# A fused attention, gated-FFN and mixture-of-experts kernel: weight blocks, clip order, score copies and filler products of the opening slots rearranged

## What is computed

```python
# attention: batch 2, 8 heads, 576 rows, head size 64
scores = scale * q @ k.T
kth = the 32nd largest of each row;  scores = where(scores >= kth, scores, -1e9)
attn = exp(scores - max) / (sum + 1e-9);  x = attn @ v          # -> 1152 x 512
# gated FFN, 512 -> 1536 -> 512
xn = x / rms(x) * rms_g;  g = xn @ w_gate
x = (g * sigmoid(g) * (xn @ w_val)) @ w_out
# experts: softmax gate over 8, argmax, capacity 288
y = relu(x_e @ w1[e]) @ w2[e];  out = gate * y
```

## Time and profile before

| | us |
|---|---|
| three executions | 663.43, 663.98, 665.63 |
| median | 663.98 |
| profiled execution, its own time | 665.63 |
| its span, first to last instruction | 663.8 |

### The profile page before, as it was taken

The page is one execution under the profiler, slowest core; times in us unless marked ns, Lnnn a source line. Parts: engine busy times, 40 slices in busy tenths (PEclk is TensorE's granted clock), DMA queues, the critical chain, the costliest instruction groups (busy, mean ns, idle before and its releaser), DMA issues.

```text
span 663.8 us, 11121 instructions
## 1 busy us (share of the span) xinstructions
PE 617.8 (93%) x3934; PEld 475.5 (72%) x3934; DVE 418.2 (63%) x915; ACT 326.3 (49%) x713; POOL 258.6 (39%) x361
## 2 busy tenths in 40 slices
PE   7777879999999999999999999999999999999994
PEld 5444555675775775775775775766769999999994
DVE  3999899799699699798898897931111110111110
ACT  3575884774865865766756756753211111111100
POOL 1284884454544544555455364462310101111101
PEclk9987999999999999999999999999999999999998
DMA  9999300000010010000000000000197767667501
GB/s 184 344 378 368 62 18 1 1 17 17 1 33 1 1 33 1 11 24 0 17 17 2 1 18 0 1 18 1 61 393 255 235 222 275 224 227 275 168 1 37
DMA packets 53070, 65.45 MB, mean 99 GB/s; under 512 B 32218, under 2 KB 32218, under 8 KB 53020
## 3 DMA queue, kind: packets, MB, share of 16 engines
q1 hardware_dynamic: 51276, 60.05, 28.2%
q0 software_dynamic: 1744, 4.76, 2.0%
HBM read 52.89 MB, written 12.30 MB: 98 GB/s over the span
## 4 chain that ended last, share of the span: by engine, by line
PE 76%; ACT 7%; POOL 4%; issue 4%; DVE 4%; SPq 3%; DMA 2%; POOLq 0%; ACTq 0%; DVEq 0%
PE ps L777 11%; PE ps L763 11%; PE ps L523 11%; PE ps L510 8%; PE ps L514 7%; PE ps L511 7%; PE ps L491 5%; PE ps L475 4%; PE ps L464 4%; PE ps L449 3%; POOL s_ring L1426 2%; ACT pt L836 2%; DMA w_loads<-in_moe_w_gate 2%; POOL hid L1369 2%; ACT z_pair L974 1%
## 5 line engine op out<-in xcount | busy, mean ns | idle before, releaser
L1426 POOL TENSOR_TENSOR s_ring<-s_ring,z_pair 128x576 f32<-128x576 f32 x72 | 100.8, 1422 | 69.5 <-ACT z_pair L974 69.5
L1249 DVE MATCH_REPLACE8 w_top<-m,w_top 128x576 f32<-128x576 f32 x144 | 105.8, 743 | 0.0
L1245 DVE MAX8 m<-w_top 128x8 f32<-128x576 f32 x144 | 101.6, 747 | 0.0
L523 PE MATMUL ps<-wo_space,hid 128*128 128x512 f32 x216 | 99.3, 593 | 0.4 <-issue 0.4
L510 PE MATMUL ps<-w_parts,x_hi 128*128 128x512 f32 x216 | 90.2, 417 | 1.8 <-DVE w_parts L1178 1.1
L511 PE MATMUL ps<-w_parts,x_hi 128*128 128x512 f32 x216 | 85.3, 395 | 0.0
L777 PE MATMUL ps<-arena,w_loads 128*128 128x168 f32 x512 | 75.8, 307 | 0.5 <-issue 0.5
L763 PE MATMUL ps<-arena,w_loads 128*128 128x168 f32 x512 | 74.3, 306 | 0.6 <-ACT arena L836 0.6
L763 PEld LDWEIGHTS ps<-arena,w_loads 128*128 128x128 f32 x512 | 73.3, 190 | 0.9 <-ACT arena L836 0.9
L777 PEld LDWEIGHTS ps<-arena,w_loads 128*128 128x128 f32 x512 | 73.2, 190 | 0.6 <-issue 0.6
L1447 POOL DMA_INDIRECT out_rows<-arena,s_ring x16 | 15.1, 941 | 147.3 <-DVE arena L1273 113.6
(11 more groups left out here) (137 smaller groups left out, 885.8 us busy)
## 6 DMA issues: line engine op xcount, KB each, us to landing
w_loads<-in_moe_w SPq DMA_DIRECT2D x16, 2048.0 KB, 9.2
dispatched_rows<-drow SPq DMA_DIRECT2D x18, 260.0 KB, 7.5
w_loads<-in_moe_w_gate SPq DMA_DIRECT2D x1, 3072.0 KB, 10.7
w_loads<-in_moe_w_val SPq DMA_DIRECT2D x1, 3072.0 KB, 18.6
wo_space<-in_moe_w_out SPq DMA_DIRECT2D x1, 3072.0 KB, 13.2
arena<-dispatched_rows SPq DMA_DIRECT2D x8, 341.2 KB
out_rows<-drow SPq DMA_DIRECT2D x9, 256.0 KB, 4.9
q_space<-in_q SPq DMA_DIRECT2D x8, 256.0 KB, 2.9
```

The source lines that it names most:

```text
L523: last = mm(blk[0], hid[:, c * P:(c + 1) * P], wo_s[:, c, :], start=(c == 0), stop=(c == CF - 1))
L1245: vec.max(m8[:, 2 * (n % 2) + a, i, :], w_top[:, a, :]).then_inc(s["top_step"], 1)
L1249: vec.match_replace(w_top[:, a, :], m8[:, 2 * (n % 2) + a, i, :], w_top[:, a, :], NEG).then_inc(s["top_step"], 1)
L1426: gp.tensor_tensor(row, row, z_pair[:, a, :], ALU.subtract).then_inc(s["lowered"], 1)
```

## The change

- **Loads.** The two weight matrices come as six blocks of 1 MB (512 columns of one matrix). Gate block 0 is issued ahead of keys of batch 1, which now go ahead of the values of batch 0; the other five follow q tile 1, with the gain among them.
- **Splits.** The high pieces start in slot 0 (pieces 0 and 1) and are spread over slots 0 to 6; low pieces follow a slot or less behind. Pieces 9 and 11 are DVE's, where 8, 9 and 10 were. FFN blocks of tile 0 wait for their own two pieces by the number of each list.
- **ACT's order in slots 0 to 4.** The two clips stand ahead of `out_columns`. The copy of the turned probabilities of a=0 stands ahead of the score copy of a=1; in slot 4 that score copy stands behind `raw_rows`. The copies of the keys of batch 1 stand near the slot's end.
- **Filler products.** `keep_running` becomes `bridge`, into `blk[1]`: 6, 4, 4 and 4 products in slots 1 to 4, behind `scores` and ahead of `turn_probs` of a=0; 2 more behind that in slot 4; one in `turn_last_pair` of tile 0. None follow `values`.
- **Tile 0's norm.** The reciprocals of the first six sums are taken on POOL in slot 3 and those of the last two behind the first scaling; before, all eight in one step in slot 4.
- **x_lo of tile 0** is made inside DVE's slot 5, between its first and second top-k round; before, behind slot 5.

```diff
--- before.py
+++ after.py
...
 START = (4, 2, 1)
-EARLY = (8, 3, 4, 3)
+EARLY = (6, 4)
 AWAKE = (1, 2)
...
 LAST = 16
-HIGH = ((1, GAMMA), (1, GAMMA), (2, GAMMA), (2, GAMMA), (4, GAMMA), (5, BETA),
-        (5, GAMMA), (5, GAMMA), (6, ALPHA), (6, GAMMA), (6, GAMMA), (7, ALPHA))
-LOW = {0: (2, ALPHA), 1: (2, ALPHA), 2: (3, ALPHA), 3: (3, ALPHA), 4: (5, BETA), 5: (5, BETA), 6: (6, ALPHA), 7: (6, BETA), 11: (7, BETA)}
-LOW_VECTOR = {8: (6, GAMMA), 9: (7, ALPHA), 10: (7, ALPHA)}
+HIGH = {0: (0, GAMMA), 1: (0, GAMMA), 2: (1, GAMMA), 3: (2, GAMMA), 4: (3, GAMMA), 5: (5, BETA),
+        6: (5, GAMMA), 7: (5, GAMMA), 8: (6, ALPHA), 9: (6, ALPHA), 10: (6, GAMMA), 11: (6, GAMMA)}
+LOW = {0: (0, GAMMA), 1: (1, ALPHA), 2: (2, ALPHA), 3: (3, ALPHA), 4: (4, ALPHA), 5: (5, BETA), 6: (6, ALPHA), 7: (6, BETA),
+       8: (6, GAMMA), 10: (7, ALPHA)}
+LOW_VECTOR = {9: (6, GAMMA), 11: (7, ALPHA)}
+HIGH_ORDER, LOW_ORDER, VECTOR_ORDER = tuple(HIGH), tuple(LOW), tuple(LOW_VECTOR)
...
         names = (
-            "q_in k_in00 k_in01 k_in02 k_in03 k_in04 k_in1 v_in0 v_in1 wg_in wv_in wo_in g_in r_in "
+            "q_in k_in00 k_in01 k_in02 k_in03 k_in04 k_in1 v_in0 v_in1 wg_in0 wg_in1 wg_in2 wv_in0 wv_in1 wv_in2 wo_in g_in r_in "
             "disp_zero out_zero id_set z_set pchain v_padded "
...
         def pieces(table, n, at):
-            return [m for m in (table if isinstance(table, dict) else range(len(table))) if table[m] == (n, at)]
+            return [m for m, place in table.items() if place == (n, at)]
+        def high_ready(m):
+            return 2 * HIGH_ORDER.index(m) + 2
...
                     q_tile(0, 0)
+            def block_in(raw, w, i, signal):
+                cols = slice(i * 512, (i + 1) * 512)
+                sp.dma_start(raw[:, :, cols], w.rearrange("(c p) f -> p c f", p=P)[:, :, cols]).then_inc(signal, 16)
+            block_in(wg_raw, w_gate, 0, s["wg_in0"])
+            key_rows(1, s["k_in1"])
             value_rows(0, s["v_in0"])
             q_tile(1, 0)
-            key_rows(1, s["k_in1"])
+            block_in(wv_raw, w_val, 0, s["wv_in0"])
+            block_in(wg_raw, w_gate, 1, s["wg_in1"])
             sp.dma_start(gain[:], rms_g.rearrange("(c p) -> p c", p=P), allow_slow_non_contiguous=True).then_inc(s["g_in"], 16)
-            sp.dma_start(wg_raw, w_gate.rearrange("(c p) f -> p c f", p=P)).then_inc(s["wg_in"], 16)
-            sp.dma_start(wv_raw, w_val.rearrange("(c p) f -> p c f", p=P)).then_inc(s["wv_in"], 16)
+            block_in(wv_raw, w_val, 1, s["wv_in1"])
+            block_in(wg_raw, w_gate, 2, s["wg_in2"])
+            block_in(wv_raw, w_val, 2, s["wv_in2"])
             sp.dma_start(wr[:], r_gate.rearrange("(c p) e -> p c e", p=P)).then_inc(s["r_in"], 16)
...
                 if t == 0:
-                    m = 4 * i + (2 if bank is blk[1] else 4)
-                    pe.wait_ge(s["w_lo_set"], sum(p < m for p in LOW))
-                    if m > min(LOW_VECTOR):
-                        pe.wait_ge(s["w_low_veced"], sum(p < m for p in LOW_VECTOR))
+                    m = 4 * i + (0 if bank is blk[1] else 2)
+                    for part in (m, m + 1):
+                        if part in LOW:
+                            pe.wait_ge(s["w_lo_set"], LOW_ORDER.index(part) + 1)
+                        else:
+                            pe.wait_ge(s["w_low_veced"], VECTOR_ORDER.index(part) + 1)
                 w_hi, w_lo = [w[:, :, i * 512:(i + 1) * 512] for w in parts]
...
                 turn(use["q", t], lambda c: q_rows[:, 2 * c:2 * c + 2, :])
-            def keep_running(count):
+            def bridge(count):
                 for _ in range(count):
-                    mm(tb[:, 0:384], ident[:], kT[0][:, 0, 0:384], start=True, stop=True)
+                    mm(blk[1][:, 0:384], ident[:], kT[0][:, 0, 0:384], start=True, stop=True)
             def stay_awake(count):
...
                         tr(last_ps, oT[:, HP - 1, :], ident[:]).then_inc(s["col_full"], 1)
+                if t == 0:
+                    bridge(1)
                 pe.wait_ge(s["normed"], 2 * t + 2)
...
                         turn_q(next_tile(n))
-                    if g == 0:
-                        keep_running(EARLY[0])
+                    if 0 <= g < HP:
+                        pe.wait_ge(s["k_acted"], KC - 1)
+                        if g > 0:
+                            pe.wait_ge(s["k1_copied"], min(2 * g, KC))
+                        bridge(EARLY[g > 0])
                     if probs:
                         turn_probs(g, 0)
+                    if g == HP - 1:
+                        bridge(2)
                     for i in (2 * n - 2, 2 * n - 1):
...
                     values(g)
-                    if g < HP - 1:
-                        if g > 0:
-                            pe.wait_ge(s["t_free"], use["q", 1] + 1)
-                        keep_running(EARLY[g + 1])
                 turn_first_rows(n)
...
                 raw, hi, _, half, cols = split_piece(m)
-                if m == 0:
-                    act.wait_ge(s["wg_in"], 16)
-                if m == 2:
-                    act.wait_ge(s["wv_in"], 16)
+                act.wait_ge(s[("wg_in", "wv_in")[m // 2 % 2] + str(m // 4)], 16)
                 for c in half:
...
                 if t >= 2:
-                    act.wait_ge(s["den_step"], 2 * t - 2)
+                    act.wait_ge(s["den_step"], 2 * t)
                 row = s_ring[:, g % SR, a, :]
...
                     dense(n, GAMMA)
+                elif n <= HP:
+                    if here:
+                        marks(g, 0)
+                        marks(g, 1)
+                        if g > 0:
+                            out_columns(g - 1)
+                        probs(g, 0)
+                    score_rows(n + 1, 0)
+                    if here:
+                        probs(g, 1)
+                        turned_probs(g, 0)
+                    if n < HP:
+                        score_rows(n + 1, 1)
+                    if here:
+                        turned_probs(g, 1)
+                        turned_probs(g, 2)
+                    t = due(n, GAMMA, XA)
+                    if t is not None:
+                        raw_rows(t)
+                    if n == HP:
+                        score_rows(n + 1, 1)
+                    if next_tile(n) is not None:
+                        q_columns(next_tile(n))
+                    for i in (2 * n - 2, 2 * n - 1):
+                        if 0 <= i < KC:
+                            act.wait_ge(s["k_turned"], KC + i + 1)
+                            keys(1, i, blk[i % 2]).then_inc(s["k1_copied"], 1)
+                    dense(n, GAMMA)
                 else:
...
                         turned_probs(g, 0)
-                    for i in (2 * n - 2, 2 * n - 1):
-                        if 0 <= i < KC:
-                            act.wait_ge(s["k_turned"], KC + i + 1)
-                            keys(1, i, blk[i % 2]).then_inc(s["k1_copied"], 1)
                     dense(n, BETA)
...
                 vec.scalar_tensor_tensor(out=hb, in0=hb, scalar=1.0, in1=blk[1], op0=ALU.add, op1=ALU.mult).then_inc(s["silu_done"], 1)
-            def low_part(n):
+            def low_part(n, first=False):
                 t = due(n, ALPHA, XB)
-                if t is not None:
+                if t is not None and first == (t == 0):
                     dve.wait_ge(s["x_hi_set"], CD * (t + 1))
...
                     raw, hi, lo, half, cols = split_piece(m)
-                    dve.wait_ge(s["w_hi_set"], 2 * m + 2)
+                    dve.wait_ge(s["w_hi_set"], high_ready(m))
                     vec.tensor_tensor(lo[:, half[0]:half[1] + 1, cols], raw[:, half[0]:half[1] + 1, cols],
...
                         beside(n - 1, GAMMA)
+                low_part(n, True)
                 for i in (1, 2):
...
                     raw, hi, lo, half, cols = split_piece(m)
-                    pool.wait_ge(s["w_hi_set"], 2 * m + 2)
+                    pool.wait_ge(s["w_hi_set"], high_ready(m))
                     gp.tensor_tensor(lo[:, half[0]:half[1] + 1, cols], raw[:, half[0]:half[1] + 1, cols],
...
                                  ALU.mult).then_inc(s["normed"], 1)
-            def norm_first(t):
-                pool.wait_ge(s["masked"], (t + 1) * H)
+            def divide(t, step, h0, h1):
+                pool.wait_ge(s["masked"], t * H + h1)
                 if t > 0:
                     pool.wait_ge(s["normed"], 2 * t)
-                gp.tensor_scalar(rden[:], den[:, t % 2, :], EPS_SUM, None, ALU.add).then_inc(s["den_step"], 1)
-                pool.wait_ge(s["den_step"], 2 * t + 1)
-                gp.tensor_tensor(rden[:], rden[:], nones[:], ALU.pow).then_inc(s["den_step"], 1)
-                pool.wait_ge(s["den_step"], 2 * t + 2)
+                gp.tensor_scalar(rden[:, h0:h1], den[:, t % 2, h0:h1], EPS_SUM, None, ALU.add).then_inc(s["den_step"], 1)
+                pool.wait_ge(s["den_step"], step + 1)
```

(9 more changed lines are left out.)

## The result

| | before | changed | ratio, 95% interval |
|---|---|---|---|
| median, 11 executions each | 665.02 (662.78 to 666.90) | 670.99 (667.48 to 672.40) | 1.0084 (1.0062 to 1.0106) |
| profiled execution, its span | 665.63, 663.8 | 670.91, 669.1 | |

The change costs 0.8%, 5.6 us. The forecast was 663.6, its range ended at 666.9, and slower had a chance of 0.22: the direction was wrong and the range missed the time.

The account below looks back on a forecast made before the run. DVE's top-k bounds the opening slots, PE the repeating rest from 108.5 us. -2.1 us at full clock plus 1.7 for slow clock gave -0.4: 665.2 on the profiled execution, 663.6 on the median; range 660.3 to 666.9.

Parts of the forecast that it names:

- the clock: PE, slots 1 to 4: one half-rate stretch after a pause, covering scores, q and a third of the fillers, +1.7 us.
- the loads: Six blocks, gate block 0 first: they cost nothing, or 2 us if a value load is late.
- the low pieces: DVE makes two, not three, at 2.5 + 2.1 = 4.6 us: 2.0 us off its chain.
- Fillers on the ring: Slot 2's loop through ACT, POOL and PE: turn of a=0 at 37.7 us, though it could have gone at 34.8.
- The wait for the second score row of slot 5: Score copy of a=1 in slot 4 lasts until 62.4 us; DVE wants it at 60.73 and waits 1.7.
- the 0.90 for x_hi: Slot 5: DVE reaches x_lo at 64.8 us and waits 0.9, x_hi being complete at 65.7.
- the rule that a delay goes on undiminished: Slots 2 to 4: delays pass fully to DVE, since the ring takes 9.65 us there against DVE's 9.66.
- the choice between the bounds: PE's clock cost: between nothing and +4.4 us, all of scores, q and fillers at half rate; +1.7 taken.
- the row behind the 2.17 us pause: PE in the kernel before: work behind its longest wait in slots 1 to 4 ran at full rate.
- The slower rival: Half clock from slot 1's gap on: 3.0 us in slots 1 and 2, 1.7 in slot 3 or 4; 666.6, chance 0.20.
- The PE part: From 108.5 us on the kernel repeats, PE-bound, period 48.13 us; the change touches nothing there.
- a sign of being wrong: The forecast is wrong if a period after 108 us is not 48.1 us.

Follow-up runs that it names:

- d_piece_late: The changed kernel with high pieces 2, 3 and 4 one slot later, their low parts in slots 3, 4 and 5: 666.75 us, ratio 1.0025.
- e_fillers_6: The changed kernel with 6 filler products in place of 4 in each of slots 2, 3 and 4: ratio 1.0093.
- a_fillers_back: The changed kernel with fillers put back at their old places, mostly behind `values`, 8, 3, 4, 3 into the other bank, none in slot 4: 659.50 us, ratio 0.9926.
- c_columns_first: The changed kernel with `out_columns` put back ahead of the clips, all else as changed: 659.48 us, ratio 0.9934.
- c_copies_back: The changed kernel with the score copy of a=1 ahead of the turned copy of a=0 in slots 1 to 4, as before: ratio 1.0098.
- d_columns_fillers: The changed kernel with fillers put back behind `values` and `out_columns` put back ahead of the clips: 662.47 us, ratio 0.9964.
- d_rest_only: The kernel before with only the changed loads and splits, tile 0's norm and x_lo inside slot 5: ratio 1.0006.
- c_order_fillers: The kernel before with ACT's new order in slots 0 to 4 and the fillers moved behind the scores: ratio 1.0148.

## Why the prediction failed, step by step

Four terms of the sum failed, with what they cost in the profiled execution: the clock, three slow stretches and not one (+3.0); the loads, which were put at nothing (+1.7); the low pieces (+1.9); the half clock behind the turn of group 7, which no term had (+1.4). Against them stands a start of DVE 2.1 us earlier, which nobody forecast and which is luck. A reading failed with the clock and the loads: DVE was said to have its scores in time up to slot 4, and it waits for them in slots 3 and 4.

Positions are counted from DVE's start (11.83 in the prediction, 9.77 after), since it differs by execution.

| | forecast | measured | late by | added in the slot before |
|---|---|---|---|---|
| clips of slot 2 | 19.77 | 21.43 | 1.66 | 1.66, the load |
| clips of slot 3 | 31.27 | 34.45 | 3.18 | 1.52 |
| clips of slot 4 | 40.92 | 45.84 | 4.92 | 1.74 |
| x_hi complete | 53.87 | 60.25 | 6.38 | 1.46 |

- **Fillers on the ring: right in mechanism.** The prediction put 2.9 us between the time when the turn could go and when it went; the rows show 4.80, 4.28 and 4.15, the 2.9 at half rate for part of it. The wait for the second score row of slot 5 (3.78 for 1.7) and the 0.90 for x_hi came where they were put. Not forecast were the waits of 1.42 and 2.81 in slots 3 and 4.
- **Clock: the term that was mis-sized.** One stretch, +1.7 us, was taken; there were three, in slots 2, 3 and 4. From the scores to the turn PE took 6.13, 5.50 and 5.48 us where the prediction's own pieces make 4.39, 3.89 and 3.89, so 1.7, 1.6 and 1.6 us more; the clips and x_hi behind them came 1.52, 1.74 and 1.46 later, 4.7 in all. Three pauses were forecast well (3.6, 3.4 and 2.7 us; they were 3.68, 3.97 and 2.88), and so was the rule that a delay goes on undiminished. The pause of 1.58 us in slot 4 was not in the list. What failed was the choice between the bounds: the row behind the 2.17 us pause ran at full rate and was the ground for the lower one. Each pause of the changed kernel shown above was followed by at least part of its work at half rate. The rule of the Trainium skill cited in the prediction ("TensorE: Matmul & The Clock Gate", HAM oscillation) says this, and the trace agrees at 23.11, 32.93 and 57.37 (1.03 for 0.66, 2.29 for 1.24 us) and not quite at 46.11, where the scores take 1.32. Other runs don't follow it each time. The same pauses of 3.68 and 1.58 us were followed by full rate in d_piece_late and in e_fillers_6 (PE's timelines):

```profile
23.91 0.66 PE L490 MATMUL ps<-ident,s_ring 128*128 128x128 f32 x4 [3.68 <-ACT s_ring L1001]
```

```profile
59.02 1.24 PE L479 MATMUL ps<-arena,q_cols 64*128 64x288 f32 x8 [1.58 <-ACT oT L856]
```

  So the length of the pause alone decides it neither way, and what does stays open. The slower rival put 4.7 on the clock, the size measured, and gave 666.6. That the sizes agree is luck: it had 3.0 of it in slots 1 and 2, and slot 1, though at half rate, moved nothing, since the clips of slot 2 are late by the load's 1.66 alone. It also lacked the next three points.
- **Loads: a step that failed.** "So the loads cost nothing" looked at the keys and values that are queued behind block 0, not at the value block, issued at 22.43 behind them all, for which ACT now waits ahead of the clips (SP's timeline of the changed kernel):

```profile
22.43 0.91 SPq L349 DMA_DIRECT2D w_loads<-in_moe_w_val  x1
```

  It cost 1.66 us at once. In d_piece_late, without that wait, x_lo comes 1.6 us earlier, and 0.9 of it is left at slot 8.
- **Low pieces: wrong.** Two at 2.5 + 2.1 were priced, 3.30 + 3.19 measured. The 2.50 was read as the price "beside a busy POOL", and it holds only for a meeting 0.94 us into POOL's piece. POOL's new pieces now start 0.1 (estimated: half of the 4.71 us of two) and 0.3 us ahead of both of DVE's.
- **The PE part: right until 108 us, wrong at the seam.** The period is 48.09 us from the turn of group 11 (161.99) to that of group 15, as before. But from group 7 to group 11 it is 49.59, which the prediction had named as a sign of being wrong. DVE's late slot 8 let PE wait 2.78 us for the turn of group 7, and behind it stands half clock (0.57 in 112 to 116 us): +1.4. The same shows in all the runs. From the start of slot 8 to the end of the execution it is 564.7 to 564.8 us in ten profiled executions, a_fillers_back and the kernel before among them. It is 566.0 to 566.4 in five: changed, c_columns_first, c_copies_back, d_columns_fillers, d_rest_only. They are the five in which DVE takes 3.1 us or more for each of two low pieces, and in each of them PE waited 2.74 to 2.79 us for that turn and took 3.67 us or more for the six products behind it, for 2.74. In the other three DVE had its two pieces done in 3.16 to 3.83 us, and PE didn't wait there (565.6 to 566.1). So a meeting of DVE and POOL in slots 6 and 7 is paid twice, about 2 us on DVE and 1.4 at the seam.

The account, forecast 665.2 on the profiled execution to 670.91: DVE's waits 8.91 for 2.6 and the 1.7 of clock already in the sum, +4.6 (the load's 1.66 and 3.0 of clock); low pieces +1.9; the earlier start -2.1; together 4.4 against the 4.3 by which the turn of group 7 is later than the 108.1 forecast; the half clock behind it +1.4. That is 5.8 of 5.7. The forecast of the median, 663.6, is off by another 1.65 us, the step from 665.63 to the median of three; of eleven executions the median is 665.02.

**Shown and not shown.** Shown by runs: the interaction of fillers and clips first (c_order_fillers against its two halves), that undoing either one gives back 10 to 11 us, in the case of a_fillers_back with 2.25 us of low pieces and the seam's 1.4 among them; that x_lo's place is worth some 5 us with an early x_hi (0.9926 and 1.0001); that with the other copy order the ring's delay shows in another wait. Read from profiles only: how the 11 us divide between length of the fillers, half clock and low pieces, and that the seam follows from the low pieces. Of the versions run, a_fillers_back is the fastest by its ratio (659.50 us), its interval overlapping that of c_columns_first.
